# A third buffer for queries and keys, and another order of the first loads

## The reference

```python
q_d, k_d, v_d = (a.reshape(B, H, 144, 4, 64).mean(axis=3) for a in (q, k, v))
out_d = softmax_attention(q_d, k_d, v_d)             # downsampled branch
out_up = np.repeat(out_d, 4, axis=2)
mask = np.abs(pos[:, None] - pos[None, :]) < 4       # local branch
scores = np.where(mask, scale * q @ k.T, -1e9)
out = out_up + softmax(scores) @ v
x = out.transpose(0, 2, 1, 3).reshape(2304, 512)
x = (silu(x @ w_gate) * (x @ w_val)) @ w_out         # inner width 1536
y = (relu(x @ w2_in) ** 2) @ w2_out                  # inner width 2048
```

## Time and profile before

| | us |
|---|---|
| median of three runs | 943.93 |
| lowest and highest of them | 942.46, 945.2 |
| the profiled execution, its own time | 945.5 |
| its span, first to last instruction | 943.7 |
| TensorE busy in the span | 915.8 |
| VectorE, ScalarE, GpSimd busy | 649.4, 403.7, 225.8 |
| mean granted clock of TensorE | 0.982 |

### The profile page before, as it was taken

How to read it: one execution, slowest core, us unless ns; L and a number is a source line. 1 busy time by engine, 2 the same in 40 slices (tenths; PEclk the granted TensorE clock), 3 DMA queues, 4 the chain that set the end, 5 groups by cost and what they waited for, 6 DMA issues and landing times.

```text
span 943.7 us, 17134 instructions
## 1 busy us (share of the span) xinstructions
PE 915.8 (97%) x6704; PEld 881.8 (93%) x6704; DVE 649.4 (69%) x1110; ACT 403.7 (43%) x733; POOL 225.8 (24%) x279
## 2 busy tenths in 40 slices
PE   6889999999999999999999999999999999999998
PEld 4678998998999999989999989999999999999998
DVE  6557555655287847696747598666788666778775
ACT  2445454545246443536443535232435232435231
POOL 5575454544242100231100133000323000302000
PEclk8589999999999999999999999999999999999999
DMA  6553333322231111321031121000232010211422
GB/s 198 174 175 93 104 91 103 105 68 73 81 113 49 53 34 34 96 87 49 30 108 53 60 90 67 1 18 17 82 101 71 17 51 17 79 59 54 135 68 67
DMA packets 70880, 71.36 MB, mean 76 GB/s; under 512 B 27280, under 2 KB 58000, under 8 KB 70800
## 3 DMA queue, kind: packets, MB, share of 16 engines
q1 hardware_dynamic: 68496, 65.55, 22.8%
q10 hardware_dynamic: 2304, 4.72, 1.3%
HBM read 56.10 MB, written 14.16 MB: 74 GB/s over the span
## 4 chain that ended last, share of the span: by engine, by line
PE 80%; DVE 9%; ACT 5%; issue 2%; SPq 1%; POOL 1%; DMA 0%; ACTq 0%; DVEq 0%
PE mlp_ps L929 11%; PE mlp_ps L930 10%; PE mlp_ps L931 10%; PE sc L929 5%; PE sc L930 5%; PE sc L931 5%; PE xp L930 4%; PE xp L929 4%; PE xp L931 4%; PE tr L788 3%; PE sd L929 2%; PE sd L931 2%; PE sd L930 2%; PE sc L769 2%; PE tr L929 2%
## 5 line engine op out<-in xcount | busy, mean ns | idle before, releaser
L1309 ACT ACTIVATE wh_hi<-hbuf 128x384 fp32r<-128x384 f32 x144 | 72.4, 524 | 85.4 <-DVE hbuf L1595 61.0
L689 POOL TENSOR_TENSOR w_raw<-w_raw 128x256 f32<-128x256 f32 x16 | 16.7, 1045 | 355.8 <-DMA w_raw<-w_in 355.8
L1603 DVE TENSOR_TENSOR wh_lo<-hbuf,wh_hi 128x384 fp32r<-128x384 f32 x144 | 76.0, 560 | 24.1 <-ACT wh_hi L1309 20.6
L1558 DVE TENSOR_TENSOR ring<-ring_raw,ring 128x768 fp32r<-128x768 f32 x96 | 90.3, 963 | 0.0
L1258 ACT ACTIVATE ring<-ring_raw 128x768 fp32r<-128x768 f32 x96 | 75.3, 836 | 28.9 <-DVE ring_raw L1552 28.6
L929 PE MATMUL mlp_ps<-ring,w_hi 128*128 128x384 f32 x240 | 80.6, 336 | 2.5 <-DVE vbuf L1571 1.9
L931 PE MATMUL mlp_ps<-ring,w_lo 128*128 128x384 f32 x240 | 80.2, 334 | 0.0
L930 PE MATMUL mlp_ps<-ring,w_hi 128*128 128x384 f32 x240 | 80.2, 334 | 0.0
L929 PE MATMUL mlp_ps<-wh_hi,w_hi 128*128 128x384 f32 x216 | 73.2, 339 | 2.6 <-DVE wh_lo L1603 1.5
L930 PE MATMUL mlp_ps<-wh_lo,w_hi 128*128 128x384 f32 x216 | 72.2, 334 | 0.0
L931 PE MATMUL sc<-wh_hi,w_lo 128*128 128x384 f32 x216 | 72.2, 334 | 0.0
(11 more groups left out here) (201 smaller groups left out, 2715.1 us busy)
## 6 DMA issues: line engine op xcount, KB each, us to landing
ring_raw<-x_whole SPq DMA_DIRECT2D x24, 384.0 KB, 3.6
ring_raw<-y_whole SPq DMA_DIRECT2D x24, 384.0 KB, 3.6
qk_sb<-qT SPq DMA_DIRECT2D x16, 288.0 KB, 2.9
qk_sb<-kT SPq DMA_DIRECT2D x16, 288.0 KB, 3.2
v_grp<-v SPq DMA_DIRECT2D x32, 144.0 KB
x_whole<-x_f ACTq DMA_DIRECT2D x16, 288.0 KB, 2.7
y_whole<-ypart SPq DMA_DIRECT2D x3, 1536.0 KB, 5.7
v_win<-v SPq DMA_DIRECT2D x64, 64.0 KB, 2.6
```

The lines of the kernel that those rows point to most:

```text
L689: nc.gpsimd.tensor_tensor(block(5), block(7), block(4), ALU.add).then_inc(s_usum[i], 1)
L1309: nc.scalar.activation(hi[:, f, t, :], hbuf[:, e, :], ACT.Copy).then_inc(s_shhi, 1)
L1558: nc.vector.tensor_tensor(ring[:, SLOTS[g][p], 1, :, :], whole(g, p), ring[:, SLOTS[g][p], 0, :, :].bitcast(F32), ALU.subtract).then_inc(s ...
L1603: nc.vector.tensor_tensor(lo[:, f, t, :], hbuf[:, e, :], hi[:, f, t, :].bitcast(F32), ALU.subtract)\
```

## The change

`qk_sb` gets a third place, so that pair i uses place i % 3 and its load waits for the downsampled scores of pair i - 3 instead of i - 2. SyncE's order becomes: queries and keys of pairs 0, 1 and 2, groups of pair 0, windows of pair 0, then in round n the weight unit, queries and keys of pair n + 3, windows of pair n + 1 (now in round 0 too), groups of pair n + 1. The slots load queries and keys one pair further ahead, behind the same semaphore values as before. VectorE clears the two spare columns of one more place, and TensorE waits for one more of these.

```diff
+QK_RING = 3
...
-        qk_sb = sb("qk_sb", [P, 2, 2, SEQ + 2])
+        qk_sb = sb("qk_sb", [P, QK_RING, 2, SEQ + 2])
...
-        s_qk = [sem(f"s_qk{i}") for i in range(2)]
+        s_qk = [sem(f"s_qk{i}") for i in range(QK_RING)]
...
-        ZEROED = 3
+        ZEROED = QK_RING + 1
 
         def load_qk(sp, i):
-            ring = i % 2
-            if i >= 2:
-
-                sp.wait_ge(s_sd, i - 1)
+            ring = i % QK_RING
+            if i >= QK_RING:
+
+                sp.wait_ge(s_sd, i - QK_RING + 1)
...
         def sp_round(sp, n):
             for i in ROUND_LOAD.get(n, []):
                 load_unit(sp, i)
-            load_qk(sp, n + 2)
-            if n > 0:
-                load_windows(sp, n + 1)
+            load_qk(sp, n + 3)
+            load_windows(sp, n + 1)
             if n < PAIRS:
                 load_groups(sp, n + 1)
...
             for i in pairs_in(1, g):
-                if i + 2 < NPAIR:
-                    load_qk(sp, i + 2)
+                if i + 3 < NPAIR:
+                    load_qk(sp, i + 3)
...
         def _(sp):
-            load_qk(sp, 0)
-            load_qk(sp, 1)
+            for i in range(QK_RING):
+                load_qk(sp, i)
             load_groups(sp, 0)
             load_windows(sp, 0)
-            load_windows(sp, 1)
...
         def downsample_qk(g, i):
-            ring = i % 2
+            ring = i % QK_RING
...
-            g.wait_ge(s_qk[ring], QK_LOAD * (i // 2 + 1))
+            g.wait_ge(s_qk[ring], QK_LOAD * (i // QK_RING + 1))
...
         def pe_scores_loc(pe, i):
-            ring = i % 2
+            ring = i % QK_RING
...
-            pe.wait_ge(s_qk[ring], QK_LOAD * (i // 2 + 1))
+            pe.wait_ge(s_qk[ring], QK_LOAD * (i // QK_RING + 1))
...
-            nc.vector.memset(qk_sb[:, 0, :, SEQ:SEQ + 2], 0.0).then_inc(s_zero, 1)
-            nc.vector.memset(qk_sb[:, 1, :, SEQ:SEQ + 2], 0.0).then_inc(s_zero, 1)
+            for i in range(QK_RING):
+                nc.vector.memset(qk_sb[:, i, :, SEQ:SEQ + 2], 0.0).then_inc(s_zero, 1)
```

## The result

| | before | changed |
|---|---|---|
| median of seven runs, us | 943.58 | 936.55 |
| lowest to highest | 942.46 to 946.05 | 935.12 to 939.86 |
| profiled execution, time and span | 945.5, 943.7 | 939.29, 937.5 |
| mean granted clock in it | 0.982 | 0.991 |

A forecast was written before the change was run, and what follows sets the result against it. TensorE was taken as the bound, its early attention rounds at half clock after pair 2's late load. Gains of 3.8 + 3.8 + 3.8 = 11.4 us from the median of 943.93 give 932.5 us; 8 in 10 range 929.6 to 937.6.

The forecast's parts named there:

- The wait removed, and the clock at 15.8: Pair 2's early load removes TensorE's 2.85 us wait and the clock fall near 15.8; first turns 3.8 us earlier, at 16.0.
- What the extra loads push back: SyncE's queue: later groups, windows and weight units cost nothing, as long as windows(0) have landed by 17 to 18 us.
- if the wait only moves (to windows, groups or a weight unit): Stated sign of being wrong: TensorE's removed wait reappears at another load; no size given.
- The sum 3.8 + 3.8 + 3.8: Early attention rounds: 3.8 us at the first turns, then two rounds of 7.6 instead of 11.4 us; gain 11.4 us.
- Can the other engines follow?: Rounds of 7.6 us: GpSimd, 27.58 us busy, fits; SyncE issues 6.6 us per round, with 1 us to spare.
- After about 60 us ... it moves as a block: Later work is started by signals of other work, so the whole gain of 11.4 us stays to the end.
- A: Early rounds: the clock swings by itself in small gaps; one slow round costs 3.8 us, giving 936.3; chance 0.14.
- B: Early rounds: only the wait goes, rounds stay at half clock; gain 2.85 us, 941.1; chance 0.09.
- D: Early transfers collide: windows(0) land after about 22 us, making the kernel slower; landing at 25 gives 947; chance 0.03.
- C: Early rounds: the wait is hidden anyway because DVE or GpSimd would hold them; 943.9; chance 0.05.

The follow-up runs named there:

- the repeat: The unaltered changed kernel timed and profiled again beside two later edits: median 938.28 us, ratio 0.9939 to the kernel before.
- the run that was to tell them apart: Late-high-halves kernel, with low halves of weight units 1 and 2 made by VectorE in slots 0 and 1 instead of GpSimd: median 937.2 us, ratio 0.9937.
- the kernel with the late high halves: Changed kernel, but ScalarE makes the high halves of weight units 1, 2 and 3 one round later: median 935.15 us, ratio 0.9906.

## Why the prediction was right, and where its size was off

*The wait removed, and the clock at 15.8*: right, to 0.2 us. 3.8 us were forecast at the first turns, 4.0 came.

*What the extra loads push back: "Cost of all this: nothing, as long as windows(0) have landed"*. This is the step that failed. The issue times were right to 0.2 us up to the groups of pair 1 (14.19 for 14.2), and pair 4's load was 1.5 us late. The landings were wrong: I asked only whether windows(0) come in time, and took for the slowest load the 5 us of pair 1's keys in the kernel before. Here 576 KB more stood ahead, the transfer engines were busy 0.95 or more in every stretch of 2 us from 4 to 24, and unit 1 took 8.46 us. Whoever waits for it stands in ScalarE's order in front of TensorE's turns. The forecast had named this way to be wrong ("if the wait only moves (to windows, groups or a weight unit)") and given it no price.

*The sum 3.8 + 3.8 + 3.8*: the terms measured 4.0, 4.4 and, for the third, minus 1.6, the round with the late unit being 12.99 us. So the third term was mis-sized, and the second a little small, since a full-clock round is 6.98 and not 7.6 us: what I took for the way from the downsampled scores to the next turns, 1.14 + 0.5 + 1.34 = 2.98, included a wait of 0.19 for VectorE, and was 2.54 (20.25 to 22.79); the rest of the round, for which I had 4.63 from a row that began below full clock (0.70 for 0.52 us), was 4.44.

*Can the other engines follow?* Both estimates were of mean load over the rounds. SyncE's 6.6 us of 7.6 were too low: in the repeat it took 7.94 and 8.41 us for a round. The sum counts 0.83 us for a pair's groups, which took 1.00, 1.01 and 2.13 there, and leaves out what SyncE waits for in its order: 0.9 us in the first of these rounds for TensorE, in front of the windows, and 0.87 us in the second for the single place for groups. GpSimd's busy time fits, and it was GpSimd that filled up behind the rounds all the same, I think because its work came in bunches behind late groups, with two low halves of 2.35 us on top; taking these away made VectorE the late one in the execution that was profiled.

*"After about 60 us ... it moves as a block"*: true of the first profiled execution up to 0.8 us, and wrong where the rounds were fast, as the forecast wanted them. In the first one 7.0 us at 42.14 were 6.9 at local scores of pair 7, and 6.2 at the end. In the repeat 12.9 became 10.1 over the first slots and 9.4 at the end; without the loads of units 1 to 3 12.7 became 10.2. The sum took what is won at the last turns for what is won at the end, and put at nothing a loss of 2.5 to 3.5 us there. GpSimd full and the half clock stand in the same stretches, and the run that was to tell them apart didn't, so the cause of this loss stays open, as does that of the last 0.7 us.

*Rivals.* A's time for one slow round, 936.3, is the median measured, 936.55, but not by A's mechanism: in round 2 the clock did not swing by itself in the short gaps but fell in a wait of 2.45 us that came from a load. That the two numbers agree is luck. Yet A's mechanism is there: in round 4 the clock fell behind idles of 0.95 and 0.50 us, in the changed kernel (the second turns at 43.16 take 0.86 us) as in the kernel before, and once, in the kernel with the late high halves, at the end of round 2 behind idles of 0.70 us and less. As to the rule of the Trainium skill that the prediction weighed ("TensorE: Matmul & The Clock Gate", "A second HAM failure mode"), that many small idles make the clock swing, these traces agree with it, and filling the gaps moved no median (935.15 with and without). B and D did not come. C did not either, for the first wait.

What is shown: the gain, and in the trace the wait for pair 2's load gone and the clock kept in its place; the late unit of the first profiled execution and its way through ScalarE; and that none of the edits, not even leaving three units out, has a median below 935. That an edit's own doing made another load late is not shown, since the program as it is varies as much from one execution to the next. Not tested is a second place for the groups, or the units issued from another engine's queue, though the chains of two executions run through GpSimd's sums and SyncE's queue to the late unit. What is only argued: that the spread of the changed kernel's times, 935 to 940, is the spread of these landings; two executions of one program with units late by 3.08 and by 0.30 us fit that, no more. The versions with the high halves later have lower medians than the changed kernel, by 3.1 us where they were timed side by side (935.15 against 938.28, with the fillers), but the intervals, 0.9894 to 0.9927 and 0.992 to 0.9958, overlap.

## What to carry to other kernels

When a stall is removed ahead of a stretch that then also runs faster, every load behind it has less time: go through the list of loads again with the new due times, and with landing times measured at full transfer engines, not at idle ones. Look in the issuing queue for waits: a load that waits for its buffer there delays all that stands behind it, also what has its own free buffer. And what is won at the end of one stage is the gain of the kernel only if the next stage can start earlier by as much. In an engine that works in order, an operation that waits for a load should stand behind those that others wait for. One profiled execution of a kernel whose loads arrive just in time is one draw; a second profile of the same program can show another critical path.

## What the runs showed of the hardware that was not expected

A transfer of 512 KB landed 8.46 us after its issue, with the transfer engines at 1.00 to 1.13 busy in the stretches of 2 us meanwhile; the quickest of this size, much later in the same execution, took 3.6 us. The small window transfers, whose rows are 64 values or 256 bytes long, seem to hold the engines at full share while moving little: in the kernel before, in the stretch in which many of them were under way, 165 GB/s at a share of 1.02, against 316 at 0.95 in 4 to 6:

```profile
6.00:8.00 2.00, 2.00 (x26) 1.78 (x23) 1.82 (x3) 0.00 (x0) 0.44 (x1) 1.00 1.02 165
```

An idle of 2.45 us was followed by matmuls at half speed (0.86 for 0.52 us), while one of 1.24 us, before the first local turns in the same execution, was not. But the length of one idle doesn't decide it: idles of 0.95 and 0.50 us in a row, in round 4, were followed by half speed too.
